# A three-stage kernel (linear attention, gated MLP, mixture of experts): row halves and result halves of the MLP turned by DMA, two gate steps reordered

## The reference

```python
def _moe_ref(x, w_in, w_out):             # x: 2304 x 512, from the attention
    h = x @ w_in                          # 512 x 2048
    relu6 = np.clip(h + 3.0, 0.0, 6.0)
    g = h * relu6 / 6.0
    return (g @ w_out).astype(np.float32) # 2048 x 512

def _moe2_ref(x, w_gate, w_output_gate, w1, w2):
    logits = x @ w_gate                   # 8 experts, one chosen per row
    e_idx = np.argmax(logits, axis=1)
    ...
        h = np.maximum(x[mask] @ w1[e], 0.0)
        ye = h @ w2[e]
        out[mask] = gate_w[mask, None] * eom[mask, e, None] * ye
```

## Time and profile before

| | us |
|---|---|
| median of 3 runs | 881.7 (881.26 to 883.32) |
| profiled execution | 881.79 |
| its span, first to last instruction | 880.1 |
| PE busy | 842.0 (96%) |
| DVE busy | 572.0 (65%) |
| ACT busy | 413.4 (47%) |
| POOL busy | 180.2 (20%) |
| mean granted TensorE clock | 0.993 of full speed |

### The profile page before, as it was taken

One profiled execution on the slowest core, in us unless ns is written; L12 is line 12 of the kernel. 1 busy time (PEld: TensorE's weight loads), 2 busy tenths in 40 slices (PEclk: granted clock), 3 DMA queues, 4 the chain that ended last, 5 costly groups with the idle time before them and its releaser, 6 DMA issues.

```text
span 880.1 us, 19939 instructions
## 1 busy us (share of the span) xinstructions
PE 842.0 (96%) x7258; PEld 562.5 (64%) x7259; DVE 572.0 (65%) x1200; ACT 413.4 (47%) x838; POOL 180.2 (20%) x208
## 2 busy tenths in 40 slices
PE   6999999999999999999999999999999999999994
PEld 5888788786555455455555455455777767777763
DVE  4777788886887897897897887863652444222221
ACT  5666578766556656566566566542310111111110
POOL 4444367652000001001001001001121222111100
PEclk9999999999999999999999999999999999999998
DMA  7345664543463563555555556256345762656610
GB/s 221 103 164 176 199 180 161 176 137 108 173 236 148 192 216 144 203 216 183 193 191 228 191 191 228 96 206 239 124 160 187 276 224 72 236 202 222 232 53 13
DMA packets 44885, 156.13 MB, mean 177 GB/s; under 512 B 7895, under 2 KB 12247, under 8 KB 38161
## 3 DMA queue, kind: packets, MB, share of 16 engines
q1 hardware_dynamic: 38896, 138.33, 44.2%
q0 software_dynamic: 5760, 16.80, 5.5%
q10 hardware_dynamic: 160, 0.07, 0.0%
HBM read 109.44 MB, written 47.47 MB: 178 GB/s over the span
## 4 chain that ended last, share of the span: by engine, by line
PE 70%; DVE 13%; issue 6%; ACT 5%; DMA 3%; POOL 2%; ACTq 0%; DVEq 0%; POOLq 0%
PE ps L856 15%; PE ps L845 13%; PE ps L952 12%; PE ps L940 12%; PE ps L761 4%; PE ps L706 3%; PE ps L733 3%; DVE u_mx L1443 2%; DVE relu L1526 2%; DVE arena L1231 2%; DMA arena<-split 2%; ACT arena L1054 2%; ACT arena L1159 1%; DVE arena L1470 1%; POOL arena L530 1%
## 5 line engine op out<-in xcount | busy, mean ns | idle before, releaser
L845 PE MATMUL ps<-arena,w_in_sb 128*128 128x384 f16 x1152 | 200.9, 326 | 1.3 <-issue 1.3
L856 PE MATMUL ps<-w_out_sb,arena 128*128 128x512 f16 x576 | 171.3, 379 | 5.2 <-DVE stage L1531 4.8
L845 PEld LDWEIGHTS ps<-arena,w_in_sb 128*128 128x128 f16 x1152 | 110.8, 98 | 75.1 <-issue 1.8
L1208 ACT ACTIVATE x_sb<-ps 128x512 f16<-128x512 f32 x54 | 31.6, 596 | 203.2 <-PE ps L940 177.9
L940 PE MATMUL ps<-x_sb,arena 128*128 128x128 f16 x2112 | 122.0, 219 | 4.3 <-issue 3.1
L940 PEld LDWEIGHTS ps<-x_sb,arena 128*128 128x128 f16 x2112 | 119.4, 98 | 8.5 <-issue 5.0
L952 PE MATMUL ps<-arena,x_sb 128*128 128x512 f16 x528 | 117.9, 379 | 0.0
L856 PE MATMUL ps<-w_out_sb,stage 128*128 128x512 f16 x288 | 109.1, 379 | 0.0
L1054 ACT ACTIVATE arena<-ps,arena 128x128 f32<-128x128 f32 x288 | 79.4, 382 | 55.2 <-DVE arena L1233 52.0
L1177 ACT ACTIVATE arena<-relu 128x384 f16<-128x384 f32 x96 | 50.2, 523 | 116.9 <-DVE relu L1526 115.6
L856 PEld LDWEIGHTS ps<-w_out_sb,arena 128*128 128x128 f16 x576 | 55.1, 98 | 65.5 <-issue 9.7
(11 more groups left out here) (211 smaller groups left out, 999.3 us busy)
## 6 DMA issues: line engine op xcount, KB each, us to landing
arena<-split SPq DMA_DIRECT2D x36, 1024.0 KB, 6.0
arena<-in_moe_w SPq DMA_DIRECT2D x16, 2048.0 KB, 13.4
split<-arena SPq DMA_DIRECT2D x16, 2048.0 KB, 7.4
arena<-in_qkt SPq DMA_DIRECT2D x15, 576.0 KB, 6.4
stage<-in_moe_w_in SPq DMA_DIRECT2D x16, 512.0 KB, 4.2
stage<-in_moe_w_out SPq DMA_DIRECT2D x16, 512.0 KB, 5.4
x_sb<-rows POOLq DMA_DIRECT2D x27, 257.0 KB, 3.0
arena<-in_v SPq DMA_DIRECT2D x32, 128.0 KB, 4.4
```

The source lines that it names most:

```text
L845: last = nc.tensor.matmul(ps[:, HB[f % GB], 0:BN], w_in_sb[:, lw, c, f * P:(f + 1) * P], xt[:, a, c, lx, :], start=c == 0 and lw + lx == 0 ...
L856: last = nc.tensor.matmul(ps[:, YB + r, :], g_sb[lg_][:, f % GB, r * P:(r + 1) * P], w_out_sb[:, lw, f, :], start=f == 0 and lg_ + lw == 0 ...
```

## The change

- Three DMA transposes for each block's rows x (blocks 1 to 5) and three for each block's y (blocks 0 to 4), each [128 partitions x 1024 fp16] to [128 x 8 x 128], issued on SP's queue: `turn_x(u // 3 + 1)` after the store of unit u and the load of unit u + 2 for u = 0, 3, 6, 9, 12, and `turn_y(u // 3)` likewise for u = 2, 5, 8, 11, 14. The SP loop over units is written out.
- PE's `x_transpose` stays for block 0 only and `y_transpose` for the last block only, with ACT's copies. PE waits for `xt_turned` ahead of a block and for `yt_turned` ahead of the logits; ACT's `x_hi` waits for the turns of the block before (it overwrites their source), and so does `rows_hi` for y.
- `xt` and `yt` are laid out with the half outside the 128-row chunk, as a transpose writes them.
- DVE's `gate_lo` comes straight after `gate_chunk` at f = 2 and 3 too (`SOON`).

```diff
@@ -62,8 +62,9 @@
 UW = DC * EF
 Q = UW // 4
 USTEPS = 5
-Y_AT, X_AT = 3, 10
+Y_AT = 3
 UNIT_AT = 1
+SOON = (0, 1, 2, 3, FC - 1)
 X_UP = 11
 YSTEPS = 7
 ONEHOT, ARGS, ROUTE = 6, 8, 21
...
@@ -124,7 +125,7 @@
         raw = [arena[:, a * UW:(a + 1) * UW] for a in range(2)]
         whole = arena[:].bitcast(F16)
         split_sb = whole[:, 4 * UW:6 * UW].rearrange("p (l n) -> p l n", l=2)
-        xt = whole[:, 6 * UW:6 * UW + 4 * DM * BT].rearrange("p (a c l n) -> p a c l n", a=2, c=DC, l=2)
+        xt = whole[:, 6 * UW:6 * UW + 4 * DM * BT].rearrange("p (a l c n) -> p a l c n", a=2, l=2, c=DC)
 
         w1_sb = [whole[:, 4 * a * UW:(4 * a + 2) * UW].rearrange("p (l c f) -> p l c f", l=2, c=DC) for a in range(2)]
         w2_sb = [whole[:, (4 * a + 2) * UW:(4 * a + 4) * UW].rearrange("p (l c d) -> p l c d", l=2, c=EFC) for a in range(2)]
...
@@ -159,7 +160,7 @@
         zrow = relu3[:].rearrange("p a n -> p (a n)")[:, 0:XW // 2]
         g_sb = (whole[:, 6 * UW + 4 * DM * BT:6 * UW + 4 * DM * BT + GB * BN].rearrange("p (a n) -> p a n", a=GB),
                 stage_all.bitcast(F16)[:, 6 * DM:6 * DM + GB * BN].rearrange("p (a n) -> p a n", a=GB))
-        yt = sb("yt", [P, DC, 2, BN], F16)
+        yt = sb("yt", [P, 2, DC, BN], F16)
         w_mx = sb("w_mx", [P, 2, 8])
         v_mx = sb("v_mx", [P, PAIRS])
         s_red = sb("s_red", [P, 4])
...
@@ -436,13 +439,34 @@
             sp.wait_ge(tails_moved, 32)
             sp.dma_start(x_sb[0:TAIL, MAIN + 1, :], x_sb[0:TAIL, MAIN + 2, :]).then_inc(tails_moved, 16)
             load_unit(0, 1, 1)
-            with sp.Fori(0, UNITS // 2 - 1) as i:
-                for a in range(2):
-                    store_unit(i * 2 + a, i, a)
-                    load_unit(i + 1, a, a)
-            store_unit(UNITS - 2, E - 1, 0)
-            store_unit(UNITS - 1, E - 1, 1)
-
+            def turn_x(n):
+
+                sp.wait_ge(xs_hi, n + 1)
+                sp.wait_ge(xs_lo, n + 1)
+                if n > 1:
+                    sp.wait_ge(h_done, (n - 1) * FC)
+                for r in range(BT):
+                    sp.dma_start_transpose(xt[:, n % 2].rearrange("p l c n -> p (l c) n")[:, :, r * P:(r + 1) * P],
+                                           xs[:, r].rearrange("p l d -> p (l d)")).then_inc(xt_turned, 16)
+
+            def turn_y(n):
+
+                sp.wait_ge(y_hi, n * BT + BT)
+                sp.wait_ge(y_lo, n + 1)
+                if n > 0:
+                    sp.wait_ge(logits_done, n)
+                for r in range(BT):
+                    sp.dma_start_transpose(yt.rearrange("p l c n -> p (l c) n")[:, :, r * P:(r + 1) * P],
+                                           yrow[:, r, 0:2 * DM]).then_inc(yt_turned, 16)
+
+            for u in range(UNITS):
+                store_unit(u, u // 2, u % 2)
+                if u + 2 < UNITS:
+                    load_unit(u // 2 + 1, u % 2, u % 2)
+                if u % 3 == 2:
+                    turn_y(u // 3)
+                if u % 3 == 0 and u // 3 + 1 < BLOCKS:
+                    turn_x(u // 3 + 1)
 
             def load_expert(k, e, a, m, half):
 
...
@@ -664,23 +688,18 @@
             def t_bank(b):
                 return ps[:, b, :].bitcast(F16)
 
-            def x_transpose(n, c, b):
+            def x_transpose(c, b):
 
                 if c == 0:
-                    if isinstance(n, int) and n == 0:
-                        pe.wait_ge(consts_made, 2)
-                    pe.wait_ge(xs_hi, n + 1)
-                    pe.wait_ge(xs_lo, n + 1)
-                    if not isinstance(n, int) or n > 1:
-                        pe.wait_ge(yt_ready, n * 4 - 4)
-                elif not isinstance(n, int) or n > 0:
-                    pe.wait_ge(xt_ready, n * 4 + c)
+                    pe.wait_ge(consts_made, 2)
+                    pe.wait_ge(xs_hi, 1)
+                    pe.wait_ge(xs_lo, 1)
                 elif c == 3:
                     pe.wait_ge(xt_ready, 1)
                 for l in range(2):
                     for r in range(BT):
                         o = 512 * l + r * P
-                        last = nc.tensor.transpose(t_bank(b)[:, o:o + P], (xs0 if isinstance(n, int) and n == 0 else xs)[:, r, l, c * P:(c + 1) * P], ident16[:])
+                        last = nc.tensor.transpose(t_bank(b)[:, o:o + P], xs0[:, r, l, c * P:(c + 1) * P], ident16[:])
                 last.then_inc(x_transposed, 1)
 
             def projections(u, a, g):
...
@@ -842,7 +861,7 @@
                     pe.wait_ge(prod_ready, before(n, f))
                 for c in range(DC):
                     for lw, lx in PARTS:
-                        last = nc.tensor.matmul(ps[:, HB[f % GB], 0:BN], w_in_sb[:, lw, c, f * P:(f + 1) * P], xt[:, a, c, lx, :],
+                        last = nc.tensor.matmul(ps[:, HB[f % GB], 0:BN], w_in_sb[:, lw, c, f * P:(f + 1) * P], xt[:, a, lx, c, :],
                                                 start=c == 0 and lw + lx == 0, stop=c == DC - 1 and lw == 1)
                 last.then_inc(h_done, 1)
 
...
@@ -862,8 +881,6 @@
                 if c == 0:
                     pe.wait_ge(y_hi, n * BT + BT)
                     pe.wait_ge(y_lo, n + 1)
-                elif not isinstance(n, int) or n < BLOCKS - 1:
-                    pe.wait_ge(yt_ready, n * 4 + c)
                 for l in range(2):
                     for r in range(BT):
                         o = 512 * l + r * P
...
@@ -873,12 +890,15 @@
 
             def y_logits(n):
 
-                pe.wait_ge(yt_ready, n * 4 + 4)
+                if isinstance(n, int) and n == BLOCKS - 1:
+                    pe.wait_ge(yt_ready, DC)
+                else:
+                    pe.wait_ge(yt_turned, n * (16 * BT) + 16 * BT)
                 pe.wait_ge(route, n * ROUTE + 1)
                 for r in range(BT):
                     for c in range(DC):
                         for ly, lw in PARTS:
-                            last = nc.tensor.matmul(ps[:, LB, r * 2 * E:(r + 1) * 2 * E], yt[:, c, ly, r * P:(r + 1) * P], wg_sb[:, lw, c, :],
+                            last = nc.tensor.matmul(ps[:, LB, r * 2 * E:(r + 1) * 2 * E], yt[:, ly, c, r * P:(r + 1) * P], wg_sb[:, lw, c, :],
                                                     start=c == 0 and ly + lw == 0, stop=c == DC - 1 and ly == 1)
                 last.then_inc(logits_done, 1)
 
...
@@ -889,9 +909,11 @@
                 nc.tensor.matmul(ps[:, LB, 192:192 + BT * E], ones[:], rhs, start=True, stop=True).then_inc(ranks_done, 1)
 
             def mlp_block(n, a, post, more=True, ahead=0):
-                pe.wait_ge(xt_ready, n * 4 + 4)
                 first = isinstance(n, int) and n == 0
-                if first:
+                if not first:
+                    pe.wait_ge(xt_turned, n * (16 * BT))
+                else:
+                    pe.wait_ge(xt_ready, DC)
 
                     pe.wait_ge(piece_hi, PAIRS // 2 - 1)
                     pe.wait_ge(piece_hi_out, PAIRS // 2 - 1)
...
@@ -912,14 +934,10 @@
                         for s in range(2):
                             slot_transposes(s, s, 1, (XB, LB)[s])
                     output(n, f)
-                    if post and Y_AT <= f + ahead // 2 < Y_AT + DC:
-                        y_transpose(n - 1, f + ahead // 2 - Y_AT, XB)
                     if post and f == Y_AT + 5 - ahead:
                         y_logits(n - 1)
                     if post and f == Y_AT + 7 - ahead:
                         ranks(n - 1)
-                    if more and X_AT <= f < X_AT + DC:
-                        x_transpose(n + 1, f - X_AT, XB)
 
             def slot_transposes(s, a, turn, bank=None):
                 bank = a if bank is None else bank
...
@@ -1074,7 +1092,8 @@
                     act.wait_ge(scale_step, X_UP)
                 else:
                     act.wait_ge(piece_lo, PAIRS // 2)
-                    act.wait_ge(x_transposed, n * 4)
+                    if not isinstance(n, int) or n > 1:
+                        act.wait_ge(xt_turned, n * (16 * BT) - 16 * BT)
                     act.wait_ge(tails_moved, 48)
                 buf = xs0 if isinstance(n, int) and n == 0 else xs
                 nc.scalar.activation(buf[:, :, 0, :], x_sb[:, bass.ds(n * BT, BT), :], ACT.Copy,
...
@@ -1141,6 +1160,7 @@
                 act.wait_ge(row_step, n * YSTEPS + 5)
                 if not isinstance(n, int) or n > 0:
                     act.wait_ge(scattered, n * (16 * BT))
+                    act.wait_ge(yt_turned, n * (16 * BT))
                 for r in range(BT):
                     nc.scalar.activation(yrow[:, r, 0:DM], ysb[:, r, :], ACT.Copy, scale=y_up[:, r:r + 1]).then_inc(y_hi, 1)
 
...
@@ -1182,14 +1202,10 @@
                         unit_hi(n * 3 + k, (odd + k) % 2, 0)
                     if 0 <= k < units and j == 4:
                         unit_hi(n * 3 + k, (odd + k) % 2, 2)
-                    if post and Y_AT + 2 <= f + ahead // 2 < Y_AT + 2 + DC:
```

(29 more changed lines are left out.)

## The result

| | before | after |
|---|---|---|
| median (lowest to highest), us, 4 runs each on one chip | 882.16 (881.26 to 883.32) | 869.06 (867.54 to 870.67) |
| profiled execution, us | 881.79 | 867.54 |
| its span, us | 880.1 | 865.8 |
| mean granted TensorE clock | 0.993 | 0.996 |

The ratio is 0.985, with a 95% interval of 0.983 to 0.987: the changed kernel is 13.1 us faster. 869.06 was measured where 872.7 was forecast; both lie inside A's range of 867 to 877. Of the 14.3 us in the span, 9.7 are the MLP's own, 0.5 were there when it began, and 4.0 came after it.

A forecast was written before the change was run, and what follows sets the result against it. PE was taken to set the MLP's length, with VectorE next; 1.5 + 4 x 1.45 + 1.8 = 9.1 us off the profiled 881.79 us gave 872.7 us, range 862 to 895.

The forecast's parts named there:

- A's range: Whole kernel: transposes hidden, VectorE and its hand-overs to ACT give most of the gain back; 867 to 877 us, chance 0.58.
- PE bounds the MLP, but VectorE is next: MLP blocks of 68.9 us: PE alone would need 63.6 without transposes and waits; VectorE's gapless run at f = 10 to 14 forbids it.
- 22.9 us: Upper end of the gain on PE: x transposes 6.7, y transposes 6.7, wait for yt 4.7, wait before `output(2)` 4.8 us.
- Rival B: MLP: PE keeps what is removed, up to 22.9 us, blocks near 64 us; kernel 859 to 867 us, chance 0.12.
- Rival E: MLP: an idle VectorE at f = 2 and 3 costs as much as freed PE gains; 879 to 884 us, chance 0.07.
- By blocks: MLP gain split by block: 1.5 us in block 0, 1.45 in each of blocks 1 to 4, 1.8 in block 5.
- `gate_lo` sooner: VectorE at f = 2 and 3: wait before `output(2)` gone, new PE waits of 1.55 us at f = 5, 1.3 at f = 15.
- Transposes on SP's queue at no cost: SP's queue: each turn takes 4.5 us, about 6.5 with landing, hidden in free gaps of 7.8 and 6.6 us; cost 0.
- 9.5 us of cover: SP's queue: a turn may take about 9.5 us, gap plus the store's spare time, before anything waits.
- C's 9 us: SP's queue: transposes outgrow their gaps, each us over 9.5 a turn costing about 9 us over all blocks; slower, chance 0.15.
- D: SP's queue: transposes run one after another, 25 us for three, the queue becomes the bound; +117, 990 us, chance 0.08.
- they move along: Slot phase after the MLP: starts earlier by the MLP's gain; weight loads, waited for 1.2 us once, move with the slot work.

The follow-up runs named there:

- e7: Changed kernel with gate_lo placed between two pieces of other work at f = 0, 1 and 2, last at f = 3 to 14: 858.94 us, 0.971 of before.
- e11: The changed kernel run again, unaltered, on the chip of the variants: 867.86 us, with 258.1 us in the phase after the MLP.
- e3: Kernel before with only the rows x turned by DMA, y on TensorE, gate order as before: 881.88 us, 0.996 of before.
- e4: Kernel before with only y turned by DMA, x on TensorE, gate order as before: 876.01 us, 0.990 of before.

## Why the prediction was right, point by point

- **PE bounds the MLP, but VectorE is next.** Right. 22.9 us were removed or aimed at on PE and 9.7 arrived in the MLP, 9.1 forecast; VectorE's share of the chain nearly doubled. Rival B would have needed blocks near 64 us, which no run has; 64.8 came only when the order was changed (e7). Rival E, the even exchange, was true of neither part: turns +16.2 us, sooner gate -6.5.
- **By blocks:** block 0 gave 1.8 us (1.5 forecast), blocks 1 to 4 gave 1.46, 1.49, 1.49 and 1.48 (1.45), block 5 gave 1.97 (1.8).
- **`gate_lo` sooner:** no wait at f = 2 and 3, 0.25 us at f = 4 (0.1 forecast), 1.38 at f = 5 (1.55), 1.14 at f = 15 (1.3), nine waits of over 1 us ("roughly nine"). The sum put the sooner low halves and the transposes together and never asked what either does alone. Had it done so for the turns with the old order, it would have found the better kernel: the wait it moved from f = 2 to f = 5 cost more at its new place, as the text itself said ("moved and grows").
- **Transposes on SP's queue at no cost:** right. 3.4 to 5.5 us a turn, where 4.5 was taken; ACT waits once for a store, for 0.4 us, and nobody for a turn. The 9.5 us of cover were a good bound: doubled turns fit but for one wait, tripled ones don't; C's 9 us for each us over 9.5 would be 9 x (3 x 4.4 - 9.5) = 33 us for these, and 23 were measured. D fell: 24 tiles of 128x128 took 3.4 to 5.5 us. The figure of 1309 ns in the Trainium skill, "VectorE: DVE Perf Modes", section "The three transpose paths", isn't borne out as a rate: a tile took some 0.2 us. The 261 GB/s of the Trainium skill, "DMA: Bandwidth & Descriptors", section "Latency and other measured facts", is borne out for the dense part: the windows have 286 GB/s in the best microsecond of transposes alone and 229 in the next; over the whole turn it is 0.79 MB / 4.4 us = 180 GB/s.
- **What didn't hold:** "they move along". The phase after the MLP was not carried over unchanged but lost 4.0 us, 3.6 of it idle time of PE (4.26 to 0.66 in the table). With the 0.5 us at the MLP's start and the 0.6 by which the MLP gained more than forecast this is the distance from 872.7 to the 867.5 of the profiled execution. The 4.0 us are luck: they repeat with the program (e11), but the sum had no term for them, their cause is open, and in e3 and e4 the phase went the other way by as much.

## What to carry to other kernels

When an engine at 96% is relieved, follow the next engine through the same steps before adding up the gain, and cost each part of a change alone as well as all together: here one part gave 16 us and the other took 6.5 of them back, and without the first part the second cost 12.9. An operation that needs another engine's answer to the instruction just before it should have some work put between, neither none (0.6 us idle) nor all of it (a late hand-over): putting it between two pieces of a longer job was worth some 6 us against the old order and 12.7 against the sooner one. And a stage that an edit doesn't touch may still change by some microseconds; compare its waits in both traces before the difference is given to what the edit was made for, and set a wait marked "issue" beside the DMA landings and instruction packets just before it ends.
